# Two feed-forward layers cut into three equal units beside the attention, with their weights streamed through a ring

## The reference

```
scores = q @ k.T / 8;  cum = cumsum(max(s, 0))
scores = where(causal, -1e9, scores + min(-(cum_i - cum_j), 0))
attn   = softmax(scores);  x = attn @ v                # heads side by side: 4 x 576 x 512
h      = max(x @ w_in, 0)                              # 512 -> 1024
conv   = w[0]*h[t-1] + w[1]*h[t] + w[2]*h[t+1]         # along the tokens
x1     = (h * sigmoid(conv)) @ w_out                   # 1024 -> 512
u      = x1 + (x1.T @ U @ V).T                         # mixing of tokens, rank 32
out    = u + max(u @ w_ch1, 0) @ w_ch2                 # 512 -> 2048 -> 512
```

## Time and profile before

| what | value |
|---|---|
| median of 3 runs | 1008.86 us (1007.39 to 1009.56) |
| the profiled execution, span | 1005.3 us |
| TensorE busy, weight loads | 928.2 us (92%), 863.0 us (86%), 5627 each |
| VectorE, ScalarE, GpSimd busy | 490.6, 336.5, 142.0 us |
| DMA | 64.41 MB, q1 at 23.2% of 16 engines |
| mean granted clock of TensorE | 0.967 |

### The profile page before, as it was taken

One profiled execution on the slowest core, in us unless ns is written; L12 is line 12 of the kernel. 1 busy time (PEld: TensorE's weight loads), 2 busy tenths in 40 slices (PEclk: granted clock), 3 DMA queues, 4 the chain that ended last, 5 costly groups with the idle time before them and its releaser, 6 DMA issues.

```text
span 1005.3 us, 14953 instructions
## 1 busy us (share of the span) xinstructions
PE 928.2 (92%) x5627; PEld 863.0 (86%) x5627; DVE 490.6 (49%) x682; ACT 336.5 (33%) x590; POOL 142.0 (14%) x99
## 2 busy tenths in 40 slices
PE   2989898999889988999987889999999999999997
PEld 2767698897778977889877879999999999999997
DVE  4677868756598546895568653121122112211211
ACT  2465554544455444554424442111111011111110
POOL 3333222300133110331015200000000000000000
PEclk9997899999899998999987999999999999999999
DMA  4565532223322324232232322010010100100000
GB/s 95 155 163 132 132 75 51 64 62 84 101 66 48 85 54 121 52 73 53 73 109 75 107 107 96 1 64 1 1 64 1 39 27 1 63 1 1 32 1 32
DMA packets 54397, 64.41 MB, mean 64 GB/s; under 512 B 29300, under 2 KB 39540, under 8 KB 54328
## 3 DMA queue, kind: packets, MB, share of 16 engines
q1 hardware_dynamic: 54328, 63.43, 23.2%
HBM read 43.79 MB, written 9.58 MB: 53 GB/s over the span
## 4 chain that ended last, share of the span: by engine, by line
PE 70%; DVE 17%; issue 6%; ACT 3%; SPq 1%; POOL 1%; DMA 1%; DVEq 0%; POOLq 0%; ACTq 0%
PE psum L1120 7%; PE psum L1118 7%; PE psum L1119 7%; PE psum L1132 7%; PE psum L1134 7%; PE psum L1133 7%; PE psum L986 6%; PE psum L1010 5%; PE psum L1012 4%; PE psum L1014 4%; DVE work L791 3%; DVE neg_max L743 3%; PE psum L932 2%; DVE sums L757 2%; DVE work L794 2%
## 5 line engine op out<-in xcount | busy, mean ns | idle before, releaser
L858 DVE SCALAR_TENSOR_TENSOR r_hl<-psum,r_hl 128x384 fp32r<-128x384 f32 x96 | 53.3, 556 | 273.6 <-ACT r_hl L675 273.6
L675 ACT ACTIVATE r_hl<-psum 128x384 fp32r<-128x384 f32 x96 | 47.2, 492 | 332.7 <-PE psum L1120 326.6
L743 DVE TENSOR_REDUCE neg_max<-psum 128x1 f32<-128x512 f32 (+4 forms) x165 | 82.9, 537 | 108.6 <-PE psum L937 102.7
L986 PE MATMUL psum<-probs,va 128*128 128x320 f32 (+4 forms) x448 | 128.5, 399 | 2.4 <-ACT probs L568 2.3
L1120 PE MATMUL psum<-ur_hl,w_buf 128*128 128x384 f32 x384 | 130.2, 339 | 0.3 <-issue 0.3
L1132 PE MATMUL psum<-r_hl,weights 128*128 128x384 f32 x384 | 128.5, 335 | 1.7 <-DVE r_hl L858 1.7
L1118 PE MATMUL psum<-ur_hl,w_buf 128*128 128x384 f32 x384 | 129.6, 337 | 0.5 <-issue 0.5
L1119 PE MATMUL psum<-ur_hl,w_buf 128*128 128x384 f32 x384 | 129.8, 338 | 0.0
L1134 PE MATMUL psum<-r_hl,weights 128*128 128x384 f32 x384 | 128.5, 335 | 0.0
L1133 PE MATMUL psum<-r_hl,weights 128*128 128x384 f32 x384 | 128.3, 334 | 0.0
L502 POOL TENSOR_TENSOR klc<-kq_raw,khh 64x576 fp32r<-64x576 f32 x34 | 50.4, 1482 | 266.0 <-ACT khh L556 266.0
(11 more groups left out here) (100 smaller groups left out, 1662.6 us busy)
## 6 DMA issues: line engine op xcount, KB each, us to landing
kq_raw<-in_kq_t SPq DMA_DIRECT2D x70, 288.0 KB, 4.0
stage<-in_w_ch SPq DMA_DIRECT2D x16, 512.0 KB, 3.3
khc<-khh SPq DMA_DIRECT2D x34, 144.0 KB, 2.3
qm<-qhl SPq DMA_DIRECT2D x34, 144.0 KB, 2.5
u_scratch<-work SPq DMA_DIRECT2D x16, 288.0 KB, 3.6
u_in<-u_scratch SPq DMA_DIRECT2D x6, 768.0 KB, 4.7
out_t<-o_sb SPq DMA_DIRECT2D x24, 192.0 KB, 1.9
va<-in_v SPq DMA_DIRECT2D x34, 128.0 KB, 3.3
```

The lines of the kernel that those rows point to most:

```text
L743: dve.tensor_reduce(neg_max[:, t:t + 1], psf[:, at:at + width], AX.X, ALU.max, negate=True)\
L986: mm = pe.matmul(psf[:, O0 + i0:O0 + i1], va[i][lo:P, t, :], probs[lo:P, c, at:at + w], start=first, stop=True, skip_group_check=True)
```

## The change

The second feed-forward layer, 512 to 2048 to 512, is cut into two units of 1024 hidden columns. So there are three units of one shape (`UNITS = 3`), the first layer and two halves of the second, and all three go tile by tile: an item is half a tile, 288 tokens, with 12 matmuls in "up" and 24 in "down". The results of units 1 and 2 are added one after the other into `x1` in SBUF (`accumulate`, a new VectorE instruction for each half tile), which holds u and at last the output; u no longer goes through DRAM. `uu_hl` holds u split.

A body has one batch's whole feed-forward work beside the next batch's attention. Its plan (`plan_of`, `spread`) is: the last 4 items of the batch before, unit 0, the tail of 10 items one a step, and then units 1 and 2 without their last 4 items. In the first body 3 steps have nothing beside them. `END` holds the 4 late items of batch 2 and everything of batch 3.

The weights of a batch are 24 blocks of 1 MB (high and low part). `ring` holds four of them. In batch 0 the raw weights are loaded (`load_raw`), split by ScalarE (`weights_high`) and GpSimd (`weights_low`), and each block is stored to `w_scratch` in DRAM (`store_block`); from then on each batch loads all 24 blocks (`load_block`), each when TensorE has read the block four places before it for the last time. The splitting in `END` and the 6-block loop are gone. Beside batch 0's attention only 4 blocks are split.

```diff
-        MAIN = [("up", f, half) for f in range(FT) for half in range(2)]
-        MAIN += [("down", d, quarter) for d in range(KT) for quarter in range(4)]
-        TAIL = [("turn", t, 0) for t in range(NT + 1)] + [("mix", d, 0) for d in range(KT)]
-        FIRST_BODY = [[] for _ in range(len(ATT_STEPS) - len(MAIN))] + [[("main", n)] for n in range(len(MAIN))]
-        BODY = [[("tail", n)] for n in range(len(TAIL))] + [[("main", n)] for n in range(len(MAIN))]
+        UP = [[("up", u, f, half, 0) for f in range(FT) for half in range(2)] for u in range(UNITS)]
+        DOWN = [[("down", u, d, half, 0) for d in range(KT) for half in range(2)] for u in range(UNITS)]
+        DOWN[0][0:2] = [("down", 0, 0, half, part) for part in (1, 2) for half in range(2)]
+        BEFORE = UP[0] + DOWN[0]
+        AFTER = UP[1] + DOWN[1] + UP[2] + DOWN[2]
+        LATE = 4
+        def plan_of(late, idle):
+            before = of(1, late) + of(0, BEFORE)
+            after = of(0, AFTER[:-LATE])
+            steps = len(ATT_STEPS) - idle - len(TAIL)
+            n = -(-steps * sum(matmuls(x) for _, x in before) // sum(matmuls(x) for _, x in before + after))
+            return [[] for _ in range(idle)] + spread(before, n) + [[(0, x)] for x in TAIL] + spread(after, steps - n)
+        FIRST_BODY = plan_of([], 3)
+        BODY = plan_of(AFTER[-LATE:], 0)
+        END = [(B - 2, x, 0) for x in AFTER[-LATE:]] + [(B - 1, x, 1) for x in BEFORE + TAIL + AFTER]
-        X_SPLIT_LAST = (1, 1)
+        X_SPLIT_LAST = (0, 2)
...
+                def load_block(q):
+                    sp.wait_ge(w_stored[q % RING].sem, 16 * (UNITS * BLOCKS // RING))
+                    sp.dma_start(ring[:, q % RING, :].bitcast(F32), w_scratch[q]).then_inc(w_ready[q % RING].sem, 16)
...
+                def hidden2(b, unit, f, half, alone):
+                    mm_up.wait(act, b, (unit - 1) * 2 * FT + 2 * f + half + 1)
+                    if f == 0 and half == 0:
+                        mm_mix.wait(act, b) if unit == 1 else mm_dn.wait(act, b, (unit - 1) * 2 * KT)
+                    act.activation(y_hl[0][:, f, cols(half)], half_at(f, half, alone), ACT.Relu).then_inc(rh.sem, 1)
...
+                def hidden2_low(b, unit, f, half, alone):
+                    rh.wait(dve, b, (unit - 1) * 2 * FT + 2 * f + half + 1)
+                    dve.scalar_tensor_tensor(out=y_hl[1][:, f, cols(half)], in0=half_at(f, half, alone), scalar=0.0,
+                                             in1=y_hl[0][:, f, cols(half)].bitcast(F32), op0=ALU.max, op1=ALU.subtract)\
+                       .then_inc(rl.sem, 1)
...
+                def up2(b, unit, f, half, alone):
+                    lag, n = 1 + alone, (unit - 1) * 2 * FT
+                    if f >= lag:
+                        rl.wait(pe, b, n + 2 * (f - lag) + half + 1)
...
+                        mm = three(half_at(f, half, alone), hi[:, k, :], lo[:, k, :],
+                                   uu_hl[0][:, k, cols(half)], uu_hl[1][:, k, cols(half)], k == 0, k == KT - 1)
```

More of the change, by code:

```diff
@@ new lines, in attention_and_ffn_program, with matmuls, spread @@
+        BEFORE = UP[0] + DOWN[0]
+        AFTER = UP[1] + DOWN[1] + UP[2] + DOWN[2]
+        LATE = 4
+        def matmuls(item):
+            kind, unit, _, _, part = item
+            return 3 * (KT if kind == "up" else {0: FT, 1: FT - 2, 2: 2}[part])
+        def spread(items, steps):
+            plan, total, done = [[] for _ in range(steps)], sum(matmuls(x) for _, x in items), 0
+            for late, x in items:
+                plan[done * steps // total].append((late, x))
+                done += matmuls(x)
+            return plan
@@ new lines, in ffn_step @@
+                def ffn_step(b, item, alone):
+                    kind, unit, i, half, part = item
+                    if kind == "up" and unit == 0:
+                        hidden(b, i, half, alone)
+                        if i:
+                            y_high(b, i - 1) if half else gate(b, i - 1)
+                    if part == 1:
+                        y_high(b, FT - 1) if half else gate(b, FT - 1)
+                    if kind == "down" and unit == 0 and part != 1:
+                        x1_tile(b, i, half, alone)
@@ L639, in ffn_step @@
                     if kind == "turn":
                         x1t_high(b, i, alone) if i < NT else g_high(b)
+                    if kind == "mix":
+                        u_high(b, i)
+                    if kind == "up" and unit:
+                        hidden2(b, unit, i, half, alone)
+                    used = used_block(item)
+                    if used is not None and is_first(b) and used + RING < UNITS * BLOCKS:
+                        last_read(act, b, item)
+                        weights_high(used + RING)
@@ L696, in _ @@
[L696 to L706 removed]
+                    ffn_step(b, item, alone)
@@ new lines, in down @@
+                def down(b, d, half, part, alone):
+                    lag = 1 + alone
+                    if part != 2:
+                        if d >= lag:
+                            x1_done.wait(pe, b, 2 * (d - lag) + half + 1)
+                        else:
+                            relu.wait(pe, b, 2 * (FT - lag + d) + half + 1)
+                        if half == 0:
+                            block_ready(b, 0, KT + d)
+                    hi, lo = down_weights(0, d)
+                    for k in {0: range(FT), 1: range(FT - 2), 2: range(FT - 2, FT)}[part]:
+                        if d == 0 and half == 0:
```

678 lines of the change are left out of this document (287 added, 391 removed).

## The result

| | before | after |
|---|---|---|
| median of runs, us | 1008.12 (1003.77 to 1009.56, 4 runs) | 1064.41 (1059.60 to 1070.29, 4 runs) |
| span of the profiled run | 1005.3 | 1058.1 (own time 1059.91) |
| ratio, 95% interval | 1 | 1.0566, 1.0509 to 1.0624 |

Both kernels were timed anew, side by side. The forecast was 1025 us, 1004 to 1050. The sign was right, the size was not: the time lies 14 us above the upper end.

A forecast was written before the change was run, and what follows sets the result against it. TensorE, busy 92% of the span, was taken as the bound. Batch 0's attention 108.5, body 1 234, bodies 2 and 3 478.6 and `END` 200.6 summed to 1021.7 us, so 1025 us as median, range 1004 to 1050.

The forecast's parts named there:

- Width of the matmuls, +9.2 us: Second layer: 3072 matmuls of 288 columns at 0.1332 us replace 2304 of 384 at 0.1736, adding 9.2 us.
- Up phase, chain of 47.4 us (54.8 in body 1): Unit 0's up phase in a body: VectorE's chain outlasts TensorE's 39.2 us, leaving 8.2 us idle, 15.6 in body 1.
- the tails, 29.4: Each body's tail stretch, one item a step, stays as thin as before and takes 29.4 us.
- VectorE's chain is longer: Up phase: convolution, tanh wait and gated run serially before the next convolution, 4.7 us a tile against TensorE's 3.2 plus 0.9.
- Clock: "2 for stretches at half clock" in `END` and nothing in the bodies: Low granted TensorE clock was to cost 2 us in `END`; no term for it in the three bodies.
- The last `u_low` ahead of unit 1: 1 us.: Between tail and unit 1 in bodies 2 and 3: TensorE waits 1 us for `u_low`.
- Batch 0, -1.6 us, bounds -4 to +3: Batch 0's attention: four fewer splits against three added 1 MB stores, from 110.1 to 108.5 us.
- `END`, 200.6: Stage after the last body, late items of batch 2 and all feed-forward work of batch 3: 200.6 us.
- Evictions of half tiles at nothing: Evictions of 1.2 us hide behind 1.6 us of TensorE work; a rival had them stall TensorE, 1049 us, chance 0.10.
- the ring: Rival: weight-block transfers bind in body 1, adding 31 us, for 1056 us; chance 0.12.
- second-layer items wait for `rl`: Sign that would show the forecast wrong: second-layer items held up waiting for `rl`; no size given.
- The gaps are filled: Rival: up phases cost TensorE nothing in the three bodies, -15.6 and -16.4 us, for 993 us; chance 0.18.

The follow-up runs named there:

- e4: Changed kernel with GpSimd's `y_low` cut to 64 of 576 columns, the rest left zero: 1021.8 us, ratio 1.0132.
- e6: Changed kernel with the convolution's centre tap moved from VectorE to ScalarE, behind the relu: 1059.6 us, ratio 1.0486.
- e7: Changed kernel with small unread matmuls ahead of each batch's last `y_low` wait, in tail steps and ahead of unit 1: 1045.3 us, ratio 1.0343.
- e17: Kernel before with `y_low` moved to VectorE, between the second and third tap: 1003.6 us, ratio 0.9893.
- e3: Changed kernel with each ring load from DRAM cut to 256 of 2048 columns: 1058.2 us, ratio 1.0410.
- e15: Changed kernel with unread matmuls at waits, last `u_low` earlier, two tail items a step, `y_low` on GpSimd cut to 64 of 576 columns: 1011.6 us, ratio 1.0011.
- pairs: Changed kernel with two tail items (turn, mix) beside one attention step instead of one: 1042.9 us, ratio 1.0345.
- fillers as well: The kernel of e16 with 24 small unread matmuls ahead of each batch's last `y_low` wait: 1024.2 us, ratio 1.0104.
- e16: Changed kernel with two tail items a step, the last `u_low` earlier and all `y_low` on VectorE, no work left out: 1029.4 us, ratio 1.0150.
- e9: Changed kernel with each batch's last `u_low` issued earlier, inside the last mix item: 1049.3 us, ratio 1.0408.
- e1: Changed kernel with 56 small unread matmuls ahead of the wait for each batch's last `y_low`: 1053.1 us, ratio 1.0378.

## Why the prediction was wrong, by its steps

- *Width of the matmuls, +9.2 us.* Right in sign, mis-sized: +5.2 by a closed stream, since 0.1332 was read from 48 pairs in a stream that also had evictions to wait for. Two widths in closed streams give (0.1736 - 0.1319) / 96 = 0.43 ns a column and 7 ns for each matmul, not 12. The Trainium skill (TensorE: Matmul & The Clock Gate, "Back-to-back issue gap") gave +1.9 us by 2.5 ns a matmul, a gap that the same section states for an isolated matmul and not for a stream that loads weights for each. The rows lie between it and my ruler.
- *Up phase, chain of 47.4 us (54.8 in body 1), and the tails, 29.4.* Right: 48.6 with 8.0 us idle (8.2 predicted) and, in body 1, 54.2 with 12.2 (15.6 predicted); tails 29.3 in body 3 and 30.8 in body 1; 34.6 in body 2, where 17 us of it were at half clock. The tile's period of 4.7 us came out as 4.69 (648.76, 653.45). Its reason, "VectorE's chain is longer", holds as a circle over VectorE and ScalarE, stretched by GpSimd (e4, e6).
- *Clock: "2 for stretches at half clock" in `END` and nothing in the bodies.* This step failed, and is the largest part. From the mean clocks, time at half clock is 2 x (1 - clock) x length: 19 + 30 + 25 = 74 us in the three bodies, against 15 + 11 + 8 = 34 before (the clocks have two digits, so each is good to some 2 us). In body 3 it falls on the dense matmuls behind the two waits shown above; in body 2, 17 us of it stand in the tail, which is 5 us longer than that of body 3. If all 40 us more fell on dense matmuls they would cost 20 us, an estimate. e7 prices the clock at 13 us by the medians and 16 to 23 by the traces, most of it in the bodies. I had the row that warned: 497.0 to 513.4 stood at 0.77 and the stage behind it at 0.85, and I carried neither into the bodies, although I had 8 to 16 us of new waiting in each.
- *"The last `u_low` ahead of unit 1: 1 us."* Failed: in body 3 3.24 us for `mixed`, which stands behind maxima, casts and a query on VectorE, 1.0 for `u_low` behind the normalising (2.0 in body 2), and 1.7 for the first down item of unit 1 (L794). About 6 us in body 3, ahead of matmuls that are all dense.
- *Batch 0, -1.6 us, bounds -4 to +3.* Failed, +4.3 in one trace and +8.4 in the next. The stores of whole blocks stand in SyncE's queue with `side`, and TensorE waited 4 times, 4.6 and 6.2 us in all, for `klc<-cum_scratch`; every trace of the changed kernel and its variants has this wait in batch 0, 3.4 to 9.0 us, and none of the three of the kernel before and its variants. "Most of a head's slack" was not there. That the stores are what delays it was not tried, and the difference in length is less firm than the wait: e17, the kernel before up to there, took 120.4 us for batch 0.
- *`END`, 200.6.* Measured 200.5, but by luck in part: 20 us of it are at half clock, which can cost up to 10, where 2 us were set aside, and e7's `END` is 195.7.
- *Evictions of half tiles at nothing; the ring.* Right for the up items: unit 2's up phase has 240 matmuls in 32.60 us with no idle time; L635 takes 0.41 us and L794 0.46. The sign "second-layer items wait for `rl`" did come, at a first down item: 5.4 us in 4 waits for L794. e3 excludes the ring's loads.
- *The rivals.* "The gaps are filled" supposed that the up phase could cost nothing. e15 comes nearest, at 1012 us and with most of `y_low` left out. That is 19 above the 993 given, so this rival was over-rated even where its condition holds.

The balance outside batch 0, from traces: after 943.7 and 936.5 us, pairs 925.8, seam and `y_low` on VectorE as well 910.3, fillers as well 905.9, before 895.2. The last 10.7 us are 5.2 of width and some 5 that stay open. Body 1 is a candidate: with `y_low` on VectorE its seven tile periods still take 39.7 us, against 33.6 in body 3, and the kernel before splits no weights in its bodies. What that costs TensorE was not measured.

## What to carry to other kernels

A wait can have two prices: its length, and what stands behind it at half clock. Where a change puts dense matmuls behind a wait that used to have thin work behind it, price both, by rows of that kernel at the lower clock. And before work is taken off an engine that seems to bound a stage, draw the circle of waits through all engines: the tap moved to ScalarE took some 0.1 us off a tile where 0.55 was expected, and `y_low` moved onto the busier VectorE bought 1% in the kernel before, and here 2% on top of the pairs (1.0345 to 1.0150). And an edit that shifts items against the attention's groups changes what stands ahead of them on every engine; look at those places before the gain is put down to the edit's purpose.

## What the runs showed of the hardware

- VectorE's two-input tap took 1.88 us beside GpSimd's 576-column subtraction and 0.82 alone, in each of the four up phases, and 2.94 to 2.95 us beside GpSimd's 1024-column split (e16, body 1, three times). GpSimd's own subtraction took 1.39 us at the least and 2.05 at the most. An operation on the idle engine cost more VectorE time (1.06 us) than doing it on VectorE (0.75). By the Trainium skill (SBUF — State Buffer, "Who interferes with whom") a VectorE instruction with two inputs in SBUF shares its second read port with GpSimd; the rows agree.
- After 3.65 us of waiting, matmuls of 288 columns started 0.24 us apart, and after 3.07 us in e9 they started at 0.13 and fell to 0.24 within a microsecond. After 1.73 us, at 776.82 in after, they kept 0.13.
- A dip prevented at one place can come at the next thin one: in e1, 17 us of half clock stood in the tail of body 3, where after has none.
